# Thirty-seven small unread products in TensorE's first waits, and SyncE waiting for the last scatters

## What is computed

```python
# 1: a decayed linear attention, one state of 48x48 per head
y[:, :, t] = einsum('bhd,bhde->bhe', rt, state + u*kt (x) vt)
state = wt * state + kt (x) vt
# 2: an MLP
x = (relu(x @ w_in) ** 2) @ w_out          # 384 -> 2048 -> 384
# 3: a mixture of 8 experts, one per row, capacity 384 rows each
expert = argmax(x @ w_gate); gate = softmax value of it
out[i] = gate_i * (relu(x_i @ w1[e]) @ w2[e])   # 384 -> 1024 -> 384
```

## Time and profile before

| | us |
|---|---|
| median of 3 runs | 470.71 (470.16 to 470.87) |
| profiled execution, its own time | 468.2 |
| its span, first to last instruction | 466.2 |
| TensorE busy in the span | 440.6 (95%) |
| VectorE busy | 313.3 (67%) |
| ScalarE busy | 251.4 (54%) |
| GpSimd busy | 52.4 (11%) |
| mean granted TensorE clock | 0.988 |

### The profile page before, as it was taken

The page is one execution under the profiler, slowest core; times in us unless marked ns, Lnnn a source line. Parts: engine busy times, 40 slices in busy tenths (PEclk is TensorE's granted clock), DMA queues, the critical chain, the costliest instruction groups (busy, mean ns, idle before and its releaser), DMA issues.

```text
span 466.2 us, 15105 instructions
## 1 busy us (share of the span) xinstructions
PE 440.6 (95%) x6263; PEld 418.8 (90%) x6263; DVE 313.3 (67%) x786; ACT 251.4 (54%) x515; POOL 52.4 (11%) x64
## 2 busy tenths in 40 slices
PE   4799999999999999999999999989999789999993
PEld 3688999999999999999999999989998679899993
DVE  4988955866687767787768648566548976678410
ACT  2265765446544664456356565572548865686420
POOL 6000000000000100010001000211030423421201
PEclk9999999999999999999999999988999999999998
DMA  7717976760410131000000094524676999420000
GB/s 259 276 63 257 334 241 244 279 235 4 147 45 1 37 116 76 3 36 4 3 3 19 20 312 164 170 85 136 225 240 184 340 332 279 142 60 1 30 17 27
DMA packets 35644, 63.44 MB, mean 136 GB/s; under 512 B 3980, under 2 KB 21950, under 8 KB 35568
## 3 DMA queue, kind: packets, MB, share of 16 engines
q1 hardware_dynamic: 33264, 57.88, 36.9%
q0 software_dynamic: 2304, 4.47, 2.6%
HBM read 50.77 MB, written 14.19 MB: 139 GB/s over the span
## 4 chain that ended last, share of the span: by engine, by line
PE 83%; DVE 9%; issue 3%; ACT 2%; DMA 1%; SPq 0%; POOL 0%; DVEq 0%; POOLq 0%; ACTq 0%
PE bank L683 21%; PE bank L669 20%; PE pair L588 6%; PE bank L885 5%; PE bank L838 4%; PE pair L550 3%; PE pair L853 3%; PE bank L853 3%; PE bank L892 3%; PE pair L838 3%; DVE KRW L1153 2%; DVE AD L1172 2%; DVE W L1122 2%; PE pair L609 2%; PE pair L644 1%
## 5 line engine op out<-in xcount | busy, mean ns | idle before, releaser
L669 PE MATMUL bank<-XH,W 128*128 128x256 f32 x576 | 119.0, 283 | 0.0
L683 PE MATMUL bank<-W,GH 128*128 128x384 f32 x372 | 98.9, 347 | 0.0
L669 PEld LDWEIGHTS bank<-XH,W 128*128 128x128 f32 x576 | 94.6, 188 | 0.7
L669 PE MATMUL bank<-XL,W 128*128 128x256 f32 x288 | 80.5, 280 | 0.0
L1018 ACT ACTIVATE RB<-bank 128x256 f32<-128x256 f32 x96 | 36.7, 382 | 55.8 <-PE bank L669 55.2
L683 PEld LDWEIGHTS bank<-W,GH 128*128 128x128 f32 x372 | 62.0, 188 | 1.2
L683 PE MATMUL bank<-W,GL 128*128 128x384 f32 x186 | 62.7, 337 | 0.0
L1209 DVE TENSOR_TENSOR GL<-GG,GH 128x256 fp32r<-128x256 f32 x96 | 40.4, 421 | 28.9 <-ACT GH L924 28.4
L924 ACT ACTIVATE GH<-GG 128x256 fp32r<-128x256 f32 x96 | 40.1, 418 | 36.1 <-PE bank L683 34.4
L588 PE MATMUL pair<-KRW 48*64 48x32 f32 (+1 forms) x2304 | 46.1, 228 | 10.9 <-DMA KRW<-in_krw 5.7
L588 PEld LDWEIGHTS pair<-KRW 48*64 48x64 f32 (+1 forms) x2304 | 40.4, 142 | 17.6 <-DVE KRW L1154 6.8
(11 more groups left out here) (162 smaller groups left out, 693.7 us busy)
## 6 DMA issues: line engine op xcount, KB each, us to landing
raw<-in_moe_w SPq DMA_DIRECT2D x23, 768.0 KB, 7.6
stage<-in_moe_w SPq DMA_DIRECT2D x9, 768.0 KB, 7.6
KRW<-in_krw SPq DMA_DIRECT2D x12, 512.0 KB, 6.3
slots<-X SPq DMA_DIRECT2D x8, 579.0 KB, 5.6
VV<-in_v SPq DMA_DIRECT2D x12, 288.0 KB, 6.9
KRW<-in_krw SPq DMA_DIRECT2D x12, 256.0 KB, 6.5
stage<-in_moe_w_in SPq DMA_DIRECT2D x4, 768.0 KB, 6.9
stage<-in_moe_w_out SPq DMA_DIRECT2D x4, 768.0 KB, 7.2
```

The costliest lines, as they stand in the source:

```text
L669: last = nc.tensor.matmul(bank[4 + f % 2][:, 0:2 * P], win[wa][:, c, f * P:(f + 1) * P], xa[:, c, :], start=n == 0, stop=n == 3 * KM - 1)
L683: last = nc.tensor.matmul(bank[6 + m][:, 0:DM], ga[(NF * g + f) % G3][:, cols], wout[wa][:, f, :], start=f == 0 and n == 0, stop=f == NF - ...
```

## The change

It has two parts. TensorE gets `narrow(n)`: n products of the identity's 32 columns with themselves into a corner of bank 4 that nobody reads. 25 stand ahead of everything but behind the wait for `made`; 6 behind `diagonal(0, 1)`; 6 behind `level(0, 0, 1)`. And the wait for the landing of the last expert's scatters is taken from GpSimd's list and put at the end of SyncE's; GpSimd no longer waits for them nor frees their buffers.

```diff
@@ block.sync
                 for c in range(CH):
                     load_part(n + c)
+            for m in range(MT):
+                sp.wait_ge(scat2[m], 16 * NE)
@@ block.gpsimd
-                for m in range(MT):
-                    pool.wait_ge(scat2[m], 16 * (e + 1))
-                    pool.sem_inc(yo_free[m], 1)
-
-            for m in range(MT):
-                pool.wait_ge(scat2[m], 16 * NE)
+                if e < NE - 1:
+                    for m in range(MT):
+                        pool.wait_ge(scat2[m], 16 * (e + 1))
+                        pool.sem_inc(yo_free[m], 1)
@@ block.tensor
+            def narrow(n):
+
+                for _ in range(n):
+                    nc.tensor.matmul(bank[4][0:32, 0:32], ident[:, 0:32], ident[:, 0:32], start=True, stop=True)
+
@@ attention(i, s, late)
                     if k < NL:
                         level(n, t, k)
+                        if (n, t, k) == (0, 0, 1):
+                            narrow(6)
                     if k == 0:
                         diagonal(n, t)
+                        if (n, t) == (0, 1):
+                            narrow(6)
@@
             pe.wait_ge(made, 1)
+            narrow(25)
             pipeline(pe, body)
```

## The result

The changed kernel took 474.56 us (median of 6 runs, 472.6 to 478.37) against 469.84 for the kernel before: a ratio of 1.0117, 95% interval 1.0085 to 1.015, which is 5.5 us (4.0 to 7.0) slower; the two medians lie 4.7 apart. The forecast was 470.3, with a range from 467.6 to 473.0 and a chance of 0.29 on slower. The profiled execution of the changed kernel took 478.37, the longest of the six, with a span of 476.4 us against 466.2.

The account below looks back on a forecast made before the run. TensorE was taken to bound the kernel from 40 to 300 us, leaving head, expert seams and tail movable. Terms -1.8 + 0 + 0 + 1.0 + 0.4 = -0.4 us gave 470.3 us in plain runs, range 467.6 to 473.0.

Parts of the forecast that it names:

- The tail: End of the kernel: with the wait on SyncE, GpSimd's 3.0 us drain begins when the scatter's issue ends; -1.8 us.
- rival (d): End of the kernel: the tail doesn't move because the drain is bound to the landing; 472.1 us, chance 0.08.
- The 148 instructions as work: Head: 50 passes take 2.8 us, hidden before the first level, and the sixes hide in waits; 0, to +0.4 us.
- The clock: Head: the small products don't raise TensorE's clock early, and little would come through; 0, from -1.1 us.
- rival (b): Head: the clock rises early and no stall is exposed, -1.8-1.1; 467.8 us, chance 0.14.
- The step that failed: From 40 to 300 us: TensorE is busy 259.22 of 260 us, so only changes to its work move that stretch.
- rival (a): Head and expert 1: the padding costs nothing, queued work covers the fetch, no head stalls; -1.8, 468.9 us, chance 0.26.
- Part 4: Code behind the 148 instructions: shifted block borders cost +1.0 us at the experts and +0.4 in the head.
- The experts: Skips at L910: long branches move from experts 2 and 3 to 1 and 5; +1.4-0.4 = +1.0 us.
- The head: From 12.89 to 22.60 us: shifted borders may make fetches late; +0.4 us, from 0 to +4.0.
- rival (c): Head, 15 to 24 us: late fetches make TensorE slip by 2.2 us; +1.4 in all, 472.1 us, chance 0.20.

Follow-up runs that it names:

- e3_realign: Changed kernel with 8 of the 9 products of unread(9) replaced by 31 products of 8 columns, shifting later code a whole block; 468.9 us, ratio 1.0017.
- e6_loads_later: Changed kernel with SyncE loading the K, V and decay rows of groups 4 and 5 three MLP products later; 467.16 us, ratio 0.9959.
- e11_no_sixes: Changed kernel with later loads of groups 4 and 5, both narrow(6) replaced by 12 products of 8 columns behind unread(9); 467.64 us, ratio 0.9984.
- second profile: The changed kernel, unaltered, measured and profiled once more for the experiments; 474.04 us, ratio 1.0111.
- e8: Kernel before with 212 more instructions behind the head, small products replacing 8 of unread(9) and 4 of unread(5); 475.46 us, ratio 1.0109.
- e7: Kernel before with 84 more instructions behind the head, 25 products of 8 columns replacing 8 of unread(9); 469.91 us, ratio 1.0023.
- e12: Kernel before with SyncE's wait, 37 products of 8 columns behind a whole unread(9), and later loads of groups 4 and 5; 468.04 us, ratio 0.9982.
- e4: Kernel before with 148 more instructions behind the head, 41 products of 8 columns replacing 8 of unread(9); 478.55 us, ratio 1.0212.
- e9: Kernel before with SyncE's wait and 144 already-met wait instructions spread over the last MLP group's hidden products; 466.1 us, ratio 0.9939.
- e10: Kernel before with SyncE's wait and 37 products of 8 columns behind a whole unread(9); 476.93 us, ratio 1.017.
- e1: Kernel before with only SyncE waiting for the last scatters in GpSimd's place, no small products; 466.23 us, ratio 0.9945.
- e5: Kernel before with SyncE's wait and 88 already-met wait instructions spread over the last MLP group's hidden products; 466.46 us, ratio 0.9954.

## Why the prediction was wrong, point by point

**The tail** (-1.8) was right, mechanism and size. From TensorE's last branch record at L912 (its line of before) to the end of the span it is 10.8 us in the trace of before and 9.0 in the changed one (10.8 in each of the four profiles with GpSimd's wait, 9.0 in each of the ten with SyncE's), and the drain begins early and ends 3.0 us behind the scatter. The sign that I had written down for rival (d), a drain of 4 us or more, was badly chosen: the drain lasts 4.2 because it starts beside the scatter.

**The 148 instructions as work** (0) were right: 2.88 us for the 50 passes where 2.8 was worked out, hidden ahead of the first level. What their code moved in the head is another matter and comes below.

**The clock** (0): rival (b)'s first half came true in two of the five profiles that have the 25 products, those of the changed kernel (0.67 us for the level at 5.23), and not in e3_realign, e6_loads_later and e11_no_sixes, where the first level took 1.08. It gave nothing that shows: at 22 us, ahead of the late fetch below, VectorE is 0.67 and 0.22 us behind the kernel before. Nor does it cost the 5.5 us: the profiled execution, with the early rise, has a mean granted clock of 0.956 (before the first rise the view counts 1.00, so an early one lowers the mean), and the five others, with 0.984 to 0.992, took 472.6 to 475.45 us. By the rule cited from the Trainium skill, page TensorE: Matmul & The Clock Gate, Part 1, activity would bring the release forward; these traces agree in two of five, and the early release brought no time here.

**The step that failed** is the first one: "nothing that leaves its work alone changes that stretch", from 40 to 300 us, and with it the use made in rival (a) of the 4488 weight loads that pass there without a stop. The row was right and the conclusion wrong. The earlier trace rows says that no fetch was late with the borders where they were; it says nothing of other borders. Part 4 worked out the price of a late fetch, counted instructions per block in the head and the borders at the experts, and left out the MLP, where four level and diagonal groups are 256 instructions in 2 us, a whole block, behind a burst of loads at 0.97. With the borders of the changed kernel the fetch waits until the loads have gone. The stops of 4.01 and 1.87 us (2.45 and 1.87 in the second profile) cost more than their length, since the clock falls behind them: 8.7 and 6.9 us between 118.5 and 205.1. The experiments show it from both sides: move the border (e3, e8, and all but 0.9 us in e7) or the loads (e6, e12), and the stops go.

The Trainium skill, page Runtime: NRT & Kernel Launch, Instruction fetch mechanics, says that the cost of crossing a block is mostly hidden. That holds for the kernel before between 40 and 300 us; the changed kernel's trace has 4.01 us at a crossing in straight code, where the block before passed in 2 us and the DMA engines were full. There the measurement decides: the crossing wasn't hidden.

**The experts** (+1.0) had the right places and, by the traces, the wrong sign. Branches of 2.9 and 1.1 us at experts 1 and 5 and short ones at 2 and 3 were forecast and came. But the row between 357.7 and 414.2 goes down by 2.1 and 2.6 us in the two profiles of the changed kernel, and by 1.4 to 2.7 in e4, e6, e9, e10, e11 and e12, which have the same borders there; e1 and e3, with the borders of before, go up by 0.9 and down by 0.9. The sign is read from these profiles; the medians of e9 and e1 don't show it. Two terms were mis-sized. At expert 1 the long branch cost 0.8 us (0.76 of stop ahead of 372.76, which the view puts down to VectorE; the difference of VectorE's instructions grows by 0.7 and 0.9 there), not 1.4. At experts 2 and 3 the short ones gave 2.6 and 3.2 (the same difference goes from +14.6 at 363.7 us to +12.0 at 386.9 in the first profile, from +11.3 to +8.1 in the second), not 0.4: I had held VectorE's late split of the earlier trace rows to be a wait of its own, next in line. When TensorE's stop goes, the split comes earlier too, so it was late because of the same stop, or at least not independent of it.

**The head** (+0.4) was about right in size, and the mechanism of rival (c) is in it. TensorE's stop of 0.79 us for "issue" at 23.51 (0.81 at 23.04 in the second profile) is the sign written down for (c), and VectorE waits for that group of `level`:

```profile
24.00 0.69 DVE L1163 TENSOR_TENSOR KRW<-KRW 128x512 f32<-128x512 f32 x1 [0.77 <-PE pair L588]
```

In the kernel before the same instruction of VectorE, at 22.47, waits for nothing. From 22 to 24 us the difference to the kernel before grows by 0.7 us in both profiles of the changed kernel, by 0.25 in e3_realign and by 1.5 in e6 and e11, and by no more than 0.02 in the eight profiles of kernels without products in the head. So a late fetch in the head does cost time, a third of (c)'s 2.2 us here. Of the rest of the +1.2 and +0.8 us at 33.0 nothing can be said: kernels with nothing added there (e1, e5, e9) show -0.4 to +1.2 at this mark.

**Between 33.0 and 44.3 us** both profiles of the changed kernel lose another 2.7 and 2.0 us that the sum didn't have. TensorE waits 1.9 us there for ScalarE's relu, which stands behind ScalarE's wait for a chunk of MLP weights:

```profile
45.84 1.49 ACT L934 ACTIVATE W<-stage 128x1536 fp32r<-128x1536 f32 x1 [5.41 <-DMA stage<-in_moe_w_in]
```

The load came late. The other kernels lose 0 to 1.0 there, but for those with the clock fall. A part of it does come from the shift. SyncE issues two loads of `VV` ahead of these weights, in the changed kernel and then in the kernel before:

```profile
35.40 1.85 SPq L359 DMA_DIRECT2D VV<-in_v  x2
```

```profile
34.23 0.82 SPq L359 DMA_DIRECT2D VV<-in_v  x2
```

A block of TensorE's code is fetched beside the long issue (one fetch between 35.6 and 37.2 us); in the kernel before it falls between 36.2 and 37.8, beside a later issue. So the first weights are issued 1.0 us later. They follow the first `VV` by 2.2 to 2.5 us in all seven profiles with the shift of 148 in this place, by 1.9 in e8, and by 1.35 in the six others. Why a longer issue goes with a fetch isn't shown. Since e6, e10, e11 and e12 lose only 0.6 to 1.0 us in this row, the rest of the 2.7 and 2.0 stays open.

**In sum**, for the second profile: -1.8 (tail) +0.8 (to 33.0) +2.0 (to 44.3) +6.9 (118.5 to 205.1) +0.7 (to 357.7) -2.6 (experts) = +6.0 us, against a measured span difference of +6.1. Rival (c) had the right kind of cause, a late fetch beside busy DMA engines, and looked for it in the head alone, where it cost 0.7 us; the MLP made the loss. That (c)'s 472.1 comes nearer to the measured time than the forecast is in the main luck.

## What to carry to other kernels

Instructions that cost nothing where they stand still move the code behind them. If the list is long, look not only at branches but at each place where a whole block of instructions (here 256) passes in a few us while loads fill the DMA engines, and ask where the block borders fall after the change; a stretch without stops proves only its present borders. If such a stop shows ("issue" with no semaphore missing, DMA share near 1 ahead of it), moving the loads by a few us is a remedy that leaves the code alone: it was worth 7.1 and 8.8 us here, at one position of the borders. At another the later loads may meet another block. The fastest kernels of this study were the ones with SyncE's wait and no products ahead of the experts (466.1 to 466.5 us, 2.2 to 2.9 under the kernel before).

## What the hardware showed that I had not expected

A fetch of instructions gave way to the loads: in the first profile of the changed kernel none began between 121.5 and 134.8 us, with the DMA engines at 0.91 to 0.97 from 129 to 133.4 us, and one as the burst ended. Behind a stop of 1.87 us in TensorE the granted clock fell to half rate (0.60 in 186 to 190 us of the second profile). And which unread products stand in a stretch showed in the clock: with 8 of 9 products of 384 columns replaced by 41 of 8 columns (e4) the clock was 0.51 from 33 to 43 us, with the nine kept and 37 small ones added (e10) it stayed at 1.00. In e3, with 31 small ones for the 8, it was 1.00 as well in the one profile, so these runs give no rule for it.
